# Windowed attention ahead of two MLPs: v loaded once in blocks by parity, attends two groups at a time, the first unit's k turned in banks of its own

## The chip, the cores and the metric

The kernel runs on one core of one Trainium2 chip. The metric is the device time of one execution in microseconds (us), lower is better. The time before is 992.86 us, the median of 3 runs (991.76 to 993.39).

## The reference

Three stages follow one another. The change touches only the first, causal attention over a window of 64 positions:

```python
# q, k, v: (4, 8, 576, 64) float32
scores = scale * q @ k^T                     # scale = 1/sqrt(64)
mask = (rel >= 0) & (rel < 64)               # rel = query position - key position
attn = softmax(where(mask, scores, -1e9))
x = (attn @ v) -> (2304, 512)                # heads side by side
x = gelu-like MLP: g = h * sigmoid(1.702 h), h = x @ w_in (512x2048), g @ w_out
out = top-2 of 8 experts by a noisy gate, each relu(x @ w1) @ w2, weighted sum
```

## The kernel before, in words

**Units and groups.** A unit is two heads of one batch entry; there are 16. A unit has 9 blocks of 64 queries. Each block sees 128 keys: the 64 of the block before and its own 64. Three blocks make a group, so a unit has 3 groups and the stage 48. A loop body handles two units, that is 6 groups, numbered m = 0 to 5. The first and the last body are written out, the six between are a hardware loop. The unit's parity (`par`) picks one of two buffers of qT, kT and v_pairs; the group's parity picks one of two PSUM banks for scores (`s_ps`), turned probabilities (`pt_ps`) and output (`o_ps`).

**Engines, each with its own fixed order.** The order of work is written out by hand for each engine, and semaphores join them. For group n, TensorE (PE) issues in this order: `turn_p(n-3)`, three transposes of normalised probabilities (L1509); `score(n)`, a mask product (L1498) and three products of queries and keys (L1501), each float32 product being two instruction records; `attend(n-4)`, six 64x64 products of probabilities and v, twelve records (L1523); after m = 0 and 3 six transposes of the next unit's q, after m = 1 and 4 six of its k (L1485). K is turned in batch 2 (four tiles) and batch 3 (two tiles), q in batches 0 and 1.

VectorE (DVE) takes the maximum (L1087, `nmx`), then for the group before it the sum (L1092, `dene`) and the reciprocal (L1095, `rden`), then copies the output of group n-5 (L1103), and it copies turned q (L1078) and k (L1081). ScalarE (ACT) copies turned probabilities (L853, `probT`), takes the exponentials (L861, `prob`) and copies turned q and k (L844, L847). GpSimd (POOL) multiplies by the reciprocal (L644, `norm`), which `turn_p` waits for, and in between converts MLP weights: `high_of_w` (L649) after m = 0 and 3, `low_of_w` (L654) after m = 1 and 4. At m = 2 and 5 it has the norm alone.

**Loads.** SyncE (SP) issues all loads in one order: v of this unit (L475, L476), q of the unit after the next (L464), weights (L481), k of the unit after the next (L470, four DMAs). `v_windows` reads 17 overlapping stretches of 128 rows, so that nearly every row of v arrives twice, and a last small DMA brings the first block's own half. V of unit u waits until unit u-2 is attended (`attended`); q waits until its single buffer is turned.

**Ends.** At the start PE turns q, then k of unit 0. All four batches go into halves of banks 3 and 4, so k batch 2 waits until DVE has copied q and k batch 3 until ACT has. At the end the last three groups are drained (`turn_p`, `attend` in turn), and the MLP begins (L1571) while its first inputs are still being split.

Of the kernel before, what the change touches and what calls it, by code (L numbers as in the profile page):

```python
# [11 lines left out]
P = 128  # L12
# [11 lines left out]
BLOCKS = S // QB  # L24
GB = 3
# [60 lines left out]
def build(nc, q, k, v, w_in, w_out, w_gate, w_noise, noise, w1, w2, out):  # L86
# [6 lines left out]
    v_v = v.rearrange("b (c two) (m p) d -> (b c) p (two m) d", two=2, p=QB)  # L93
    v_windows = bass.AP(v.tensor, v.offset, [[2 * S * DH, UNITS], [DH, P], [QB * DH, 2 * BLOCKS - 1], [1, DH]])
# [6 lines left out]
    with ctx:  # L101
# [28 lines left out]
        mask = sa("mask", [P, GB, P], mybir.dt.bfloat16)  # L130
# [5 lines left out]
        kT = [sa(f"kT{i}", [P, QB + S]) for i in range(2)]  # L136
# [150 lines left out]
        tr_ps = [banks[3][:, 0:S // 2], banks[4][:, 0:S // 2], banks[3][:, 0:SPLIT], banks[4][:, 0:S - SPLIT]]  # L287

# [24 lines left out]
        attended = sem("attended")  # L313
        o_copied = sem("o_copied")
# [139 lines left out]
        def k_part(u_par, batch):  # L454

            first = tiles_of(batch)[0] * TP
            count = len(tiles_of(batch)) * TP
            return kT[u_par][:, QB + first:QB + first + count], tr_ps[batch]

        @block.sync  # L460
        def _(sp):
# [148 lines left out]
        def _(pool):  # L610
# [5 lines left out]
            nc.gpsimd.memset(v_pairs[0][0:QB, 0, :], 0.0).then_inc(consts_ready, 1)  # L616
            nc.gpsimd.memset(v_pairs[1][0:QB, 0, :], 0.0).then_inc(consts_ready, 1)
            nc.gpsimd.memset(kT[0][:, 0:QB], 0.0).then_inc(consts_ready, 1)
            nc.gpsimd.memset(kT[1][:, 0:QB], 0.0).then_inc(consts_ready, 1)
            nc.gpsimd.memset(mask[:], 0.0).then_inc(consts_ready, 1)  # L620
            nc.gpsimd.memset(ident_b[:], 0.0).then_inc(consts_ready, 1)
            pool.wait_ge(consts_ready, 8)
            nc.gpsimd.affine_select(out=ident_b[:], in_=ident_b[:], compare_op=ALU.not_equal, fill=1.0, base=0,
                                    pattern=[[-1, P]], channel_multiplier=1).then_inc(consts_ready, 1)
            pool.wait_ge(consts_ready, 9)
            for h in range(2):
                half = mask[h * QB:(h + 1) * QB, :, :]

                nc.gpsimd.affine_select(out=half, in_=half, compare_op=ALU.is_gt, fill=NEG, base=0,
                                        pattern=[[0, GB], [1, P]], channel_multiplier=-1).then_inc(consts_ready, 1)  # L630
            pool.wait_ge(consts_ready, 11)
            for h in range(2):
                half = mask[h * QB:(h + 1) * QB, :, :]
                nc.gpsimd.affine_select(out=half, in_=half, compare_op=ALU.is_ge, fill=NEG, base=QB,
                                        pattern=[[0, GB], [-1, P]], channel_multiplier=1).then_inc(consts_ready, 1)
            pool.wait_ge(consts_ready, 13)

            nc.gpsimd.memset(mask[:, 0, 0:QB], NEG).then_inc(consts_ready, 1)
# [198 lines left out]
        def _(act):  # L837
            def turned(u, par, batch):
# [6 lines left out]
                else:  # L845
                    dst, src = k_part(par, batch)
                    ins = nc.scalar.activation(dst, src, ACT.Copy)  # L847
# [17 lines left out]
            def body(i, first, last):  # L865
                for m in range(6):
# [930 lines left out]
```

## Time and profile before

| | |
|---|---|
| median of the runs | 992.86 us |
| the profiled execution: its own time | 993.39 us |
| its span | 991.7 us |
| PE busy | 970.2 us (98%) |
| DVE, ACT, POOL busy | 546.6, 438.3, 484.2 us |
| queue q1 (all loads of SP) | 185.02 MB, 62.9% of 16 DMA engines |
| attention stage | from the start to the first MLP product at 116.59 us |

The device time of an execution lies about 1.7 us above its span. The page's share of busy time is an average over three different stages. A PE matmul's end is modelled, so the step from one start to the next tells more than the busy time. All times below are us from the span's start.

### The profile page before, as it was taken

The numbers are of one execution on the slowest core, as the hardware profiler recorded it, in microseconds if no ns is written. First come the engines' busy times: TensorE is split into PE (matmuls) and PEld (weight loads), VectorE is DVE, ScalarE is ACT, GpSimd is POOL, SyncE is SP. The second block draws the span as 40 slices with busy tenths as digits, with TensorE's granted clock in tenths as the row PEclk, the third lists the DMA queues.
The fourth block names the chain that finished last, engine by engine and source line by source line (L and its number), as shares of the span: only waits on it lengthen the run. The fifth ranks groups of instructions, "written<-read, shape, count | busy, mean of one in ns | idle before, by whom it ended". The sixth has DMA issues, their size and how long they took to land.

```text
span 991.7 us, 19802 instructions
## 1 busy us (share of the span) xinstructions
PE 970.2 (98%) x5432; PEld 844.7 (85%) x5433; DVE 546.6 (55%) x1328; ACT 438.3 (44%) x1094; POOL 484.2 (49%) x564
## 2 busy tenths in 40 slices
PE   7999999999999999999999999999999999999995
PEld 6888899999999999999998788888888888888884
DVE  4667622225225233243344887676777777767762
ACT  5899843333342342342243444443444444444431
POOL 5566678756877787787927221221221221122121
PEclk9999999999999999999999999999999999999998
DMA  7999677959999999999838525888976869494211
GB/s 176 213 220 221 122 232 257 319 166 309 341 294 328 321 316 338 318 286 291 267 114 290 175 85 160 253 268 274 258 224 207 254 181 292 135 283 140 55 57 49
DMA packets 252496, 225.25 MB, mean 227 GB/s; under 512 B 84620, under 2 KB 182412, under 8 KB 252432
## 3 DMA queue, kind: packets, MB, share of 16 engines
q1 hardware_dynamic: 214352, 185.02, 62.9%
q0 software_dynamic: 9280, 28.62, 8.1%
q10 hardware_dynamic: 28800, 10.83, 5.0%
q8 instruction: 32, 0.52, 0.2%
q14 instruction: 32, 0.26, 0.1%
HBM read 140.68 MB, written 85.82 MB: 228 GB/s over the span
## 4 chain that ended last, share of the span: by engine, by line
PE 94%; DVE 2%; DMA 2%; issue 1%; SPq 1%; ACT 1%; POOL 0%; POOLq 0%; ACTq 0%
PE bank L1674 22%; PE bank L1682 21%; PE bank L1571 20%; PE bank L1590 20%; PE bank L1501 3%; PE bank L1523 2%; PE bank L1485 2%; DMA q_raw<-q 2%; PE bank L1615 2%; PE bank L1509 1%; PE bank L1607 1%; DVE hT L1255 1%; PE bank L1498 1%; SPq L476 1%; DVE he L1274 0%
## 5 line engine op out<-in xcount | busy, mean ns | idle before, releaser
L1674 PE MATMUL bank<-W,xe 128*128 (+1 forms) x960 | 226.1, 391 | 0.0
L1682 PE MATMUL bank<-W,he 128*128 (+1 forms) x960 | 224.7, 389 | 1.1 <-DVE he L1274 1.1
L1674 PEld LDWEIGHTS bank<-W,xe 128*128 128x128 f32 x960 | 181.2, 189 | 37.8
L1682 PEld LDWEIGHTS bank<-W,he 128*128 128x128 f32 x960 | 179.9, 188 | 39.0 <-issue 1.9
L1590 PE MATMUL bank<-W,gs 128*128 128x512 f32 x864 | 205.8, 392 | 0.0
L1571 PE MATMUL bank<-xs,W 128*128 128x384 f32 x768 | 197.0, 337 | 0.2 <-DVE gs L1151 0.2
L1590 PEld LDWEIGHTS bank<-W,gs 128*128 128x128 f32 x864 | 161.2, 188 | 32.0
L1255 DVE STREAM_TRANSPOSE hT<-bank 32x256 f32<-32x256 f32 x320 | 144.1, 450 | 42.1 <-PE bank L1674 37.9
L1151 DVE TENSOR_TENSOR gs<-bank,gs 128x384 fp32r<-128x384 f32 x96 | 53.5, 557 | 187.2 <-ACT gs L900 187.2
L795 POOL DMA_INDIRECT out<-y_sb,yrow x40 | 41.3, 1032 | 233.5 <-DVE y_sb L1287 224.4
L958 ACT ACTIVATE hq<-bank 32x256 f32<-32x256 f32 x320 | 119.8, 374 | 67.2 <-PE bank L1674 61.4
L1571 PEld LDWEIGHTS bank<-xs,W 128*128 128x128 f32 x768 | 138.5, 188 | 3.0 <-DVE gs L1151 0.5
L900 ACT ACTIVATE gs<-bank 128x384 fp32r<-128x384 f32 x96 | 47.2, 492 | 200.2 <-PE bank L1590 194.4
L681 POOL TENSOR_TENSOR raw<-raw,xT 128x512 fp32r<-128x512 f32 x99 | 127.9, 1292 | 8.0
L1571 PE MATMUL bank<-xT_low,W 128*128 128x384 f32 x384 | 128.8, 335 | 0.0
L1330 DVE TENSOR_TENSOR bank<-bank,gate 128x384 f32<-128x384 f32 x96 | 53.9, 561 | 79.5 <-ACT gate L989 79.4
L679 POOL CAST xT<-raw 128x512 fp32r<-128x512 f32 x99 | 60.8, 614 | 45.8 <-DMA split_weights<-xT 45.2
L948 ACT ACTIVATE xe<-xr 128x512 fp32r<-128x512 f32 x40 | 25.3, 632 | 115.2 <-DVE xr L1234 115.2
L989 ACT ACTIVATE gate<-bank 128x384 f32<-128x384 f32 x96 | 47.0, 490 | 60.4 <-PE bank L1571 56.3
L1571 PEld LDWEIGHTS bank<-xT_low,W 128*128 128x128 f32 x384 | 72.1, 188 | 0.0
L784 POOL DMA_INDIRECT part<-out,yrow x40 | 42.8, 1071 | 46.6 <-issue 42.5
L1269 DVE SCALAR_TENSOR_TENSOR he<-hT,he 128x1024 fp32r<-128x1024 f32 x34 | 41.7, 1225 | 36.3 <-ACT he L971 36.3
(185 smaller groups left out, 1034.4 us busy)
## 6 DMA issues: line engine op xcount, KB each, us to landing
W<-split_weights SPq DMA_DIRECT2D x112, 512.0 KB
raw<-moe_w SPq DMA_DIRECT2D x128, 256.0 KB, 3.7
split_weights<-raw SPq DMA_DIRECT2D x112, 256.0 KB, 4.1
split_weights<-xT SPq DMA_DIRECT2D x99, 256.0 KB, 4.2
xg<-x_by_expert ACTq DMA_DIRECT2D x160, 64.0 KB
v_pairs<-v SPq DMA_DIRECT2D x16, 544.0 KB, 4.2
q_raw<-q SPq DMA_DIRECT2D x16, 288.0 KB, 3.7
out<-zeros SPq DMA_DIRECT2D x12, 384.0 KB, 4.5
```

The lines of the kernel that those rows point to most:

```text
L679: nc.gpsimd.tensor_copy(high_w, job_raw[n % 5]).then_inc(ej_high, 1)
L681: nc.gpsimd.tensor_tensor(low_w, job_raw[n % 5], high_w.bitcast(F32), ALU.subtract).then_inc(ej_low, 1)
L900: nc.scalar.activation(gs[c % 2][:, 0], h_ps[c % 2][:, 0:TG], ACT.Copy).then_inc(g_high, 1)
L958: ins = nc.scalar.activation(hq[c * Q:(c + 1) * Q, :].rearrange("p (k q i) -> p k q i", q=2, i=Q)[:, :, q], src[q * Q:(q + 1) * Q, :, c], ...
L989: nc.scalar.activation(gate[:], h_ps[c % 2][:, 0:TG], ACT.Sigmoid, scale=1.702).then_inc(sigmoided, 1)
L1151: nc.vector.tensor_tensor(gs[c % 2][:, 1], h_ps[c % 2][:, 0:TG], gs[c % 2][:, 0].bitcast(F32), ALU.subtract).then_inc(g_low, 1)
L1255: nc.vector.transpose(dst[c * Q:(c + 1) * Q, :, q], src[q * Q:(q + 1) * Q, :, c])
L1330: nc.vector.tensor_tensor(h_ps[c % 2][:, 0:TG], h_ps[c % 2][:, 0:TG], gate[:], ALU.mult).then_inc(gated, 1)
L1571: ins = nc.tensor.matmul(h_ps[c % 2][:, 0:TG], w_in_s[:, wl, c, d], x_low(g, d) if xl else x_high(g, d), start=(d == 0 and wl + xl == 0), ...
L1590: ins = nc.tensor.matmul(y_ps[t][:], gs[c % 2][:, gl, t * P:(t + 1) * P], w_out_s[:, wl, c], start=(c == 0 and gl + wl == 0), stop=(c == F ...
L1674: ins = nc.tensor.matmul(h2_ps[par][:, f * 512:(f + 1) * 512], xe[par][:, xl, d * P:(d + 1) * P], weights(e, wl, d * FE + f * 512), start= ...
L1682: ins = nc.tensor.matmul(ye_ps[par][:], he[par][:, hl, c * P:(c + 1) * P], weights(e, wl, W1COLS + c * DM), start=(c == 0 and wl + hl == 0 ...
```

## The change

Four parts. (1) V is read once, in four DMAs for a unit: for either head the even blocks into partitions 0 to 63 and the odd blocks into partitions 64 to 127. GpSimd then makes the missing halves with two copies for each unit (`pair_v`), after the norm of the unit's third group. In the loop the load of v now follows that of q. A window's key halves now stand even block first, and the mask and kT are laid out by parity to match; k's last batch becomes two copies on DVE. (2) PE attends groups n-5 and n-4 together at odd m instead of one at every m, and the first attend of a unit waits for `v_paired`. (3) K of unit 0 is turned into banks 5 and 6, and its two waits go. (4) ScalarE's table is loaded at the start of its stream.

```diff
@@ SyncE
-                sp.dma_start(v_pairs[par][:, 1:], v_windows[u]).then_inc(v_loaded[par], 16)
-                sp.dma_start(v_pairs[par][QB:P, 0:1], v_v[u, :, 0:1]).then_inc(v_loaded[par], 16)
+                for h in range(2):
+                    sp.dma_start(v_by_head(par, slice(0, QB))[:, h, 0:EVENS], v_even[u, :, h]).then_inc(v_loaded[par], 16)
+                    sp.dma_start(v_by_head(par, slice(QB, P))[:, h, EVENS:], v_odd[u, :, h]).then_inc(v_loaded[par], 16)
...
-                load_v(u, par)
+                if last or (isinstance(i, int) and i == 0):
+                    load_v(u, par)
                 if not last:
                     load_q(u + 2)
+                if not (last or (isinstance(i, int) and i == 0)):
+                    load_v(u, par)
@@ GpSimd
+            def pair_v(i, par):
+                pool.wait_ge(normed, i * 6 + par * 3 + 3)
+                pool.wait_ge(v_loaded[par], i * 64 + 64)
+                pool.sem_inc(v_seen, 1)
+                even, odd = v_by_head(par, slice(0, QB)), v_by_head(par, slice(QB, P))
+                nc.gpsimd.tensor_copy(even[:, :, EVENS:], even[:, :, 0:ODDS]).then_inc(v_paired, 1)
+                nc.gpsimd.tensor_copy(odd[:, :, 1:EVENS], odd[:, :, EVENS:]).then_inc(v_paired, 1)
+                pool.wait_ge(v_paired, i * 4 + par * 2 + 2)
...
                     norm(i * 6 + m, m)
+                    if m % 3 == 2:
+                        pair_v(i, m // 3)
@@ ScalarE and VectorE
-                    dst, src = k_part(par, batch)
+                    for dst, src in k_parts(u, par, batch):
...
+            nc.scalar.preload_act_table(ACT.Exp)
@@ TensorE
-                if batch == 2:
+                if batch == 2 and not first_unit(u):
                     pe.wait_ge(turned_dve, u * 2 + 1)
-                if batch == 3:
+                if batch == 3 and not first_unit(u):
                     pe.wait_ge(turned_act, u * 2 + 1)
...
-                    pe.wait_ge(v_loaded[par], i * 32 + 32)
+                    pe.wait_ge(v_paired, u * 2 + 2)
...
-                    if not (first and m < 4):
+                    if m % 2 and not (first and m < 5):
+                        attend(n - 5, i if m >= 5 else i - 1, (m - 5) % 6)
                         attend(n - 4, i if m >= 4 else i - 1, (m - 4) % 6)
```

On TensorE, before, m = 0 and m = 1 of the loop body hold one attend each. In the names prob, probT, kT, qT and v_pairs the digit is the buffer, and banks 3 and 4 take the turned q.

```order
L1498 MATMUL bank0<-mask,ident_b 128x384 [waits exped]
L1501 MATMUL bank0<-kT0,qT0 128x128 x3
L1523 MATMUL bank12<-probT0,v_pairs0 64x64 [waits o_copied]
L1523 MATMUL bank12<-probT0,v_pairs0 64x64 x5
L1485 MATMUL bank3<-ident,q_raw 128x96 [waits turned_act]
L1485 MATMUL bank4<-ident,q_raw 128x96 [waits turned_dve]
L1509 MATMUL bank56<-ident,prob1 128x128 [waits p_copied,normed]
L1498 MATMUL bank12<-mask,ident_b 128x384 [waits exped]
L1501 MATMUL bank12<-kT0,qT0 128x128 x3
L1523 MATMUL bank7<-probT1,v_pairs1 64x64 [waits o_copied,p_copied,v_loaded1]
```

The same place after the change, on TensorE: one stretch without attends, then both.

```order
L1547 MATMUL bank0<-mask,ident_b 128x384 [waits exped]
L1549 MATMUL bank0<-kT0,qT0 128x128 x3
L1534 MATMUL bank3<-ident,q_raw 128x96 [waits turned_act]
L1534 MATMUL bank4<-ident,q_raw 128x96 [waits turned_dve]
L1558 MATMUL bank56<-ident,prob1 128x128 x2
L1547 MATMUL bank12<-mask,ident_b 128x384 [waits exped]
L1549 MATMUL bank12<-kT0,qT0 128x128 x3
L1572 MATMUL bank12<-probT0,v_pairs0 64x64 [waits o_copied]
L1572 MATMUL bank12<-probT0,v_pairs0 64x64 x5
L1572 MATMUL bank7<-probT1,v_pairs1 64x64 [waits o_copied,p_copied,v_paired]
```

The attend of the odd unit's first group (v_pairs1) stands at the same m as before, but it now waits for GpSimd's copies, and the attend ahead of it came down from m = 0.

On GpSimd, before, the end of the loop body has three norms and no more than the weights' work between them.

```order
L644 TENSOR_TENSOR prob1<-prob1,rden 128x384 [waits exped,inverted]
L654 ISA [waits raw_high]
L654 TENSOR_TENSOR W<-w_raw1,W 128x512
L644 TENSOR_TENSOR prob2<-prob2,rden 128x384 [waits exped,inverted]
L664 COMPARE_AND_BRANCH
```

The same place after the change, on GpSimd:

```order
L678 TENSOR_TENSOR prob1<-prob1,rden 128x384 [waits exped,inverted]
L688 ISA [waits raw_high]
L688 TENSOR_TENSOR W<-w_raw1,W 128x512
L678 TENSOR_TENSOR prob2<-prob2,rden 128x384 [waits exped,inverted]
L696 COPY v_pairs1<-v_pairs1 64x2x256 [waits normed,v_loaded1]
L697 COPY v_pairs1<-v_pairs1 64x2x256
L710 REGISTER_ALU [waits v_paired]
L710 COMPARE_AND_BRANCH
```

The two copies stand behind the norm of m = 5, and the next body's first norm stands behind them.

## Rows read from the trace of the kernel before

**Rows 1.** Busy time by stretch: us, engines, granted clock, DMA share, GB/s.
```profile
50.00:75.00 25.00, 24.81 (x306) 22.43 (x305) 17.80 (x59) 22.48 (x92) 15.98 (x20) 1.00 1.04 221
```

**Rows 2.** Chain that ended last, 21 to 51 us: start, us, what.
```profile
21.46 0.48 PE bank L1509 x3
...
43.98 0.65 PE bank L1485 x6
...
45.12 0.67 PE bank L1501 x6
45.79 0.50 PE bank L1523 x12
46.29 0.64 PE bank L1485 x6
46.93 0.33 PE bank L1509 x3
...
50.40 0.68 PE bank L1485 x6
```

**Rows 3.** PE alone, one narrow window: start, us to the last record's end, count.
```profile
45.94 0.35 PE L1523 MATMUL bank<-probT,v_pairs 128*64 128x64 f32 x6
```

**Rows 4.** Who waits for whom, 25 to 105 us: total, times, longest.
```profile
PE bank L1485 <- DMA q_raw<-q: 1.7, 4, 0.8
```

**Rows 5.** The same for SP's DMA queue, 0 to 130 us.
```profile
SPq L475 <- PE bank L1523: 12.0, 12, 3.3
```

**Rows 6.** All engines in order of time, a piece of one loop body.
```profile
45.30 0.87 ACT L844 ACTIVATE qT<-bank 64x288 f32<-64x288 f32 x2
...
46.19 0.49 ACT L853 ACTIVATE probT<-bank 128x384 f32<-128x384 f32 x1
...
48.90 0.33 PE L1498 MATMUL bank<-mask,ident_b 128*128 128x384 bf16 x1
50.02 0.56 DVE L1087 TENSOR_REDUCE nmx<-bank 128x3 f32<-128x384 f32 x1 [0.53 <-PE bank L1501]
50.50 0.15 DVE L1092 TENSOR_REDUCE dene<-den 128x3 f32<-128x6 f32 x1
51.06 0.83 POOL L644 TENSOR_TENSOR prob<-prob,rden 128x384 f32<-128x384 f32 x1
```

**Rows 7.** The conversion L649, 20 to 106 us: ns min/median/max.
```profile
L649 POOL CAST W<-w_raw x14: 609/612/614, 20.1 to 105.8; 128x512 f32 x12, 128x512 fp32r<-128x512 f32 x2
```

**Rows 8.** All engines in order of time, the start.
```profile
3.02 1.10 POOL L629 TENSOR_SCALAR_AFFINE_SELECT mask<-mask 64x384 bf16<-64x384 bf16 x2
4.27 1.10 POOL L634 TENSOR_SCALAR_AFFINE_SELECT mask<-mask 64x384 bf16<-64x384 bf16 x2
4.42 1.19 PE L1485 MATMUL bank<-ident,q_raw 96*128 96x96 f32 x6 [4.42 <-DMA q_raw<-q]
5.70 1.28 ACT L844 ACT_TABLE_LOAD   x1 [5.54 <-PE bank L1485]
...
8.58 0.36 DVE L1081 COPY kT<-bank 128x192 f32<-128x192 f32 x1 [2.40 <-PE bank L1485]
9.08 0.48 PE L1498 MATMUL bank<-mask,ident_b 128*128 128x384 bf16 x1 [0.54 <-DVE kT L1081]
```

**Rows 9.** All engines in order of time, the end of the stage.
```profile
112.24 0.55 PE L1509 MATMUL bank<-ident,prob 128*128 128x128 f32 x3
112.44 0.37 ACT L861 ACTIVATE prob<-bank,nmx 128x128 f32<-128x128 f32 x1 [0.27 <-DVE nmx L1087]
114.08 0.83 POOL L644 TENSOR_TENSOR prob<-prob,rden 128x384 f32<-128x384 f32 x1 [0.49 <-DVE rden L1095]
114.39 0.57 PE L1523 MATMUL bank<-probT,v_pairs 128*64 128x64 f32 x12 [0.20 <-DVE xT L1103]
114.96 0.55 PE L1509 MATMUL bank<-ident,prob 128*128 128x128 f32 x3
116.59 0.62 PE L1571 MATMUL bank<-xs,W 128*128 128x384 f32 x2
```

More of the change, by code:

```diff
@@ L135, in build @@
         qT = [sa(f"qT{i}", [P, BLOCKS, 2, QB]) for i in range(2)]
-        kT = [sa(f"kT{i}", [P, QB + S]) for i in range(2)]
+        kT = [sa(f"kT{i}", [P, 2, EVENS, QB]) for i in range(2)]
         v_pairs = [sa(f"v_pairs{i}", [P, 2 * BLOCKS, DH]) for i in range(2)]
@@ L313, in build @@
         attended = sem("attended")
+        v_paired = sem("v_paired")
+        v_seen = sem("v_seen")
+        v_zero = sem("v_zero")
         o_copied = sem("o_copied")
@@ L452, in q_parts, with first_unit, turned_bank, k_parts @@
                        tr_ps[h][e * DH:(e + 1) * DH].rearrange("c (b p) -> c b p", b=BLOCKS))
[L454 to L458, printed above, removed]
+        def first_unit(u):
+            return isinstance(u, int) and u == 0
+        def turned_bank(u, batch):
+            return (first_tr_ps if first_unit(u) else tr_ps)[batch]
+        def k_parts(u, u_par, batch):
+            src = turned_bank(u, batch)
+            if batch == 2:
+                half = SPLIT // QB // 2
+                yield kT[u_par][:, :, 0:half], src.rearrange("c (j e k) -> c e j k", e=2, k=QB)
+            else:
+                blocks = src.rearrange("c (n k) -> c n k", k=QB)
+                first = SPLIT // QB
+                yield kT[u_par][:, 0, first // 2:EVENS], blocks[:, 0:BLOCKS - first:2]
+                yield kT[u_par][:, 1, first // 2:ODDS], blocks[:, 1:BLOCKS - first:2]
+        def k_window(u_par, qb):
+            view = kT[u_par][:].rearrange("c e j k -> c (e j) k")
+            j = qb // 2
+            other = EVENS + (j if qb % 2 else (j - 1) % EVENS)
+            return view[:, j:other + 1:other - j]
+        def v_slot(h, qb):
+            return h * BLOCKS + (EVENS if qb % 2 else 0) + qb // 2
+        def v_by_head(u_par, rows):
+            return v_pairs[u_par][rows].rearrange("p (h s) d -> p h s d", h=2)
         @block.sync
@@ L626, in _ @@
             for h in range(2):
[L627 to L635, printed above, removed]
@@ L636, in _ @@
-            pool.wait_ge(consts_ready, 13)
-            nc.gpsimd.memset(mask[:, 0, 0:QB], NEG).then_inc(consts_ready, 1)
+                half = mask[h * QB:(h + 1) * QB].rearrange("q s (b k) -> q (s b) k", k=QB)
+                for at in (0, 3):
+                    nc.gpsimd.affine_select(out=half[:, at::4], in_=half[:, at::4], compare_op=ALU.is_ge, fill=NEG, base=0,
+                                            pattern=[[0, 3 - at // 3], [-1, QB]], channel_multiplier=1).then_inc(consts_ready, 1)
@@ L640, in norm @@
+                for at in (2, 5):
+                    nc.gpsimd.affine_select(out=half[:, at::4], in_=half[:, at::4], compare_op=ALU.is_gt, fill=NEG, base=0,
+                                            pattern=[[0, 2], [1, QB]], channel_multiplier=-1).then_inc(consts_ready, 1)
+            pool.wait_ge(consts_ready, 15)
+            nc.gpsimd.memset(mask[:, 0, QB:P], NEG).then_inc(consts_ready, 1)
             def norm(n, m):
@@ L1079, in turned @@
                 else:
-                    dst, src = k_part(par, batch)
-                    ins = nc.vector.tensor_copy(dst, src)
+                    for dst, src in k_parts(u, par, batch):
+                        ins = nc.vector.tensor_copy(dst, src)
                 ins.then_inc(turned_dve, 1)
@@ L1127, in _ @@
             ins.then_inc(q_zero, 1)
+            for par in range(2):
+                nc.vector.memset(v_by_head(par, slice(QB, P))[:, :, 0], 0.0).then_inc(v_zero, 1)
             dve.wait_ge(q_zero, 1)
@@ L1496, in score @@
                 bank = s_ps[(par * 3 + g) % 2]
-                allowed = mask[:] if g == 0 else mask[:, 1:2, :].to_broadcast([P, GB, P])
+                allowed = mask[:, g:g + GB]
                 nc.tensor.matmul(bank[:, 0:GB * P], ident_b[:], allowed, start=True, stop=False)
                 for b in range(GB):
-                    at = (g * GB + b) * QB
-                    ins = nc.tensor.matmul(bank[:, b * P:(b + 1) * P], qT[par][:, g * GB + b].rearrange("c h q -> c (h q)"),
-                                           kT[par][:, at:at + P], start=False, stop=(b == GB - 1))
+                    ins = nc.tensor.matmul(bank[:, b * P:(b + 1) * P].rearrange("q (n k) -> q n k", n=2),
+                                           qT[par][:, g * GB + b].rearrange("c h q -> c (h q)"),
+                                           k_window(par, g * GB + b), start=False, stop=(b == GB - 1))
                 ins.then_inc(scored, 1)
```

28 lines of the change are left out of this document (15 added, 13 removed).

## The prediction

> **What bounds the kernel now.** I read the page first: the change touches only the attention stage, the first 116.6 us of the span, where the first MLP product starts [rows 9]. Then the busy time by stretch. From 50 to 75 us TensorE is busy for 24.81 of 25 us at full granted clock, ScalarE for 22.48, VectorE for 17.80, GpSimd for 15.98, and the DMA share is 1.04 [rows 1]. Two resources look full, so the chain and the waits must tell them apart. The chain is TensorE instruction after instruction: the reader should see that each piece begins where the last one ends, score 0.67, attend 0.50, six transposes 0.65, three transposes 0.33 [rows 2]. In 80 us TensorE waited 1.7 us for q, four times, 0.8 at most [rows 4], while SyncE waited 12.0 us for TensorE's attends before it could load v [rows 5]. So the loads are paced by TensorE, and TensorE bounds, with the loads just behind.
>
> One step from one turning of q to the next is 43.98 to 50.40, 6.42 us [rows 2], a body of two units 12.85. From the first `turn_p` of body 1 (21.46 [rows 2]) to the first one of the drain (112.24 [rows 9]) are 90.8 us; the last body lacks one turning of q and one of k, 1.15 by the chain's 0.65 and 0.50, so a body took (90.8 + 1.15) / 7 = 13.13. The 0.28 above 12.85 are waits, those for q above all.
>
> **Attends in pairs.** Three transposes take 0.48 behind an attend at 21.46 [rows 2] and 0.33 behind six transposes [rows 2]: leaving an attend costs 0.15. Twelve records of an attend take 0.50 [rows 2], but in the stream six of them end after 0.35 with 0.22 of that the last one's length [rows 3], so a step is about 0.027 and twelve need 0.31 to 0.35: entering costs 0.15 too. A second attend right behind the first thus costs 0.35, and a pair saves 0.30. Three pairs in a body save 0.90: 12.85 becomes 11.95 if nothing else is late. This is work off the critical engine, so it counts in full unless a wait eats it. The waits for q should go as well, since v is now 1152 rows of 256 bytes for a unit instead of 2240, of some 4530 in all four loads.
>
> **The new wait, in the loop.** What is late next? GpSimd's pair of copies. The attend of an odd unit's first group stands at m = 1, the second of its pair, and waits for `v_paired`; the copies stand behind the norm of m = 5 of the body before. Take the mask product of m = 0 as zero. Before, that norm began 51.06 - 48.90 = 2.16 later, because VectorE sums only after the maximum of m = 0 (50.02, 50.50) [rows 6]. It takes 0.83, so it ends at 2.99. The copies wait for it; a GpSimd instruction that waits for GpSimd's own last one began 0.15 late (3.02 + 1.10 = 4.12, next 4.27) [rows 8]. No row shows a copy of 64 partitions by 512 elements. The nearest is the conversion of 128 by 512, 0.61 [rows 7]; two, slightly overlapped, 1.2. With 0.05 for the semaphore v is ready at 4.4. TensorE would come to that attend at 0.16 + 0.67 + 0.50 (q) + 0.33 + 0.16 + 0.67 + 0.50 (first attend) = 2.99. It waits 1.4 us, and behind it in its queue stand the turning of k, the next `turn_p` and the next score, so all is late by that. The bounds of one copy: 0.31 if half the partitions took half the time of rows 7, and 1.11 if it ran at the norm's rate (0.83 for 384 elements [rows 6]); over two copies and seven bodies and the drain, 16 copies, that is -4.8 and +8.0 us. I take 0.61, the same operation with the same elements for each partition.
>
> The even unit's pair stands behind the norm of m = 2, and its attend is the first of m = 5, almost three steps later; I find it ready some 0.7 before and cost it at nothing. GpSimd has the room: 15.98 of 25 is 8.4 in a body, and 2.4 are added. The norm of m = 0 and m = 3 starts behind the copies, and `turn_p` wants it three groups later; also nothing, but with little over.
>
> The Trainium skill speaks to this cover: its page "GPSIMD Engine Reference", section 1, says that GpSimd shares its SBUF interfaces with VectorE and contends with it in some of its modes. Fourteen conversions took 609 to 614 ns while VectorE was busy for 71% of the time [rows 1, 7], so this trace shows no such stretch; by the rule the copies would be longer and the time higher.
>
> **A smaller wait.** At odd m the copy of probT on ScalarE now waits for the first attend of the same m, which ends about 1.5 behind the mask (0.16 + 0.67 + 0.57 [rows 2, 9] and the entry). Copy (0.4 of its 0.49), exponentials (1.2) and q (0.87) [rows 6] bring ScalarE's q to 4.0; TensorE wants it for k batch 3 at m = 4, at 0.83 + 0.85 + 0.65 + 0.33 + 0.83 + 0.33 = 3.8. Cost 0.2 for a body, between 0 and 0.4. At m = 1 the long wait covers it. The second DVE copy of k (some 0.25 for a unit) lies in VectorE's idle third.
>
> So a body is 11.95 + 1.4 + 0.2 = 13.55, and the seven, less 1.25 for what the last lacks (0.2 of it the small wait, the rest the two turnings without a full exit), 93.6 against 90.8: +2.8.
>
> **The start.** Before, ScalarE loads its table only when the first q is turned (5.70, 1.28 us), k waits for q's copies, and the first mask product starts at 9.08 [rows 8]. Now TensorE turns q until 5.6 and k right behind at the same pace, 0.2 each, until 6.8. VectorE copies k in two pieces until 7.5 (the whole took 0.36 [rows 8]), ScalarE's q and k end near 7.0. The mask product starts at 7.5, 1.5 earlier. The mask's constants took 1.10 for two pieces of 384 [rows 8]; eight pieces of 128 to 192 are ready between 5.5 and 7.5. The next q and k are loaded no earlier by as much, so I take 1.35, between 0.8 and 1.7.
>
> **The drain.** The last pair of copies stands behind the very last norm, and TensorE wants it one attend earlier, before `turn_p(47)`. From `turn_p(45)` (112.24) the norm began at 1.84, the attend at 2.15 and the MLP at 4.35 [rows 9]. Exponentials and `turn_p(45)` both move by about 0.3, so the norm still starts near 1.8 and ends at 2.6; copies until 3.95; the attend starts at 4.0, then `turn_p(47)` and the rest as before. That is +1.85, between +1.2 and +2.9 by the copies' bounds.
>
> **The sum.** -1.35 + 2.8 + 1.85 = +3.3 us. Against the profiled execution's 993.39 this is 996.7, against the median 996.2; I say 996.4.
>
> **Rivals.** (A) The copies are hidden: GpSimd has 9 idle us for every 25 [rows 1], and if the norm ran earlier than I think, all of the pairing's gain stays. Bodies 7 x 11.95 - 1.05 = 82.6, that is -8.2, with the start and no loss in the drain: -9.5, 983.5. Against it: the norm cannot start before VectorE's sum, 1.6 behind the mask [rows 6], and so v not before 3.8. Chance 0.10.
> (B) The loads bound the stage: share 1.04 [rows 1]. Then the waits of the loop are theirs, 24% fewer packets take 13.13 to 10.0, below TensorE's 11.95, and TensorE waits for copies as in A only where its lead allows; about 985. SyncE's 12.0 us of waiting [rows 5] speaks against it. Chance 0.04. The Trainium skill would back it: "DMA: Bandwidth & Descriptors", Specifications, wants 512 bytes for a transfer at line rate, and v's and k's rows here have 256; but the trace has TensorE wait only 1.7 us of 80, so the rule, true or not, prices nothing large.
> (C) The other side of my size: the copies run at the two-input rate. +8.0 more, 1004.4, slower. It decides from some 0.9 us a copy, where also GpSimd (8.4 + 3.6 + waits of 13.5) begins to hold `turn_p`. Chance 0.06.
> (D) The copies are near 0.35: the wait is 0.85, the sum -0.9 at 0.35 each, 992; or TensorE wastes less than I count at one of 23 pairs. Within 0.2% or faster. Chance 0.22. A late k (for the even unit v, weights and k stand behind the attend of m = 1; 0.8 was the longest wait for a load [rows 4]) would fall beside the wait for v and not add to it.
>
> The forecast has 0.58. A measurement of this kernel can tell 0.2% (2 us) from no change. Faster: A, B and 0.09 of D, 0.23. Same: 0.13 of D and 0.06 of the forecast, 0.19. Slower: the rest of the forecast and C, 0.58. The range is 989.5 to 1001; A, B and C lie outside.
>
> **What would show it.** `v_paired` from GpSimd's L697 as the longest releaser of TensorE's attends (L1572), about 1.4 at m = 1 of each body, none at m = 5; the copies 0.61 each; 7.5 for the first mask product; six transposes at m = 0 straight behind the score, 12 records at a second attend in 0.35; a DMA share near 0.8 and no wait for q. I am wrong if TensorE's attends never wait for GpSimd, or if the body is under 13.

## The result: 1001.48 us, 0.9% slower

The changed kernel takes 1001.48 us (median of 5 runs, 1000.35 to 1001.88), the kernel before 992.38 (991.76 to 993.39) beside it: ratio 1.0089, interval 1.0079 to 1.0100. The forecast was 996.4 with a range to 1001.0, so the direction was right and the size was not: +9.1 us instead of +4.

The profiled execution has a span of 1000.2 us against 991.7. The first MLP product starts at 125.25 instead of 116.59 [rows 9], 8.66 later, and what lies behind it takes 874.95 instead of 875.1. The loss lies in the attention stage, as far as these two traces show it.

### The profile page after: what moved, and what is told of

Same layout as the page of the kernel before. It is cut to its first block, busy times and chain, and to the rows that moved or that the text cites. A ratio compares the mean times of both kernels' runs of the same rounds, so it can differ in the third digit from the quotient of the medians.

```text
span 1000.2 us, 19972 instructions
## 1 busy us (share of the span) xinstructions
PE 967.8 (97%) x5432; PEld 844.7 (84%) x5433; DVE 546.4 (55%) x1346; ACT 439.4 (44%) x1094; POOL 502.9 (50%) x598
## 4 chain that ended last, share of the span: by engine, by line
PE 91%; DVE 2%; issue 2%; POOL 1%; SPq 1%; DMA 1%; ACT 1%; POOLq 0%; DVEq 0%; ACTq 0%
PE bank L1725 21%; PE bank L1733 21%; PE bank L1622 20%; PE bank L1641 20%; PE bank L1549 2%; PE bank L1572 2%; PE bank L1666 2%; PE bank L1534 1%; PE bank L1558 1%; PE bank L1658 1%; DVE hT L1304 1%; POOL prob L678 1%; DMA k_raw<-k 1%; PE bank L1547 1%; POOL v_pairs L697 0%
```

## The profile after

First the start of the stage, all engines in order of time (start, us, instruction, in brackets the wait before it and who ended it).

```profile
4.40 1.19 PE L1534 MATMUL bank<-ident,q_raw 96*128 96x96 f32 x6 [4.40 <-DMA q_raw<-q]
5.38 1.17 PE L1534 MATMUL bank<-ident,k_raw 96*128 96x96 f32 x6
...
6.59 0.42 DVE L1128 COPY kT<-bank 128x128 f32<-128x128 f32 x2 [0.43 <-PE bank L1534]
...
7.37 0.48 PE L1547 MATMUL bank<-mask,ident_b 128*128 128x384 bf16 x1 [0.82 <-ACT kT L893]
```

K is turned straight behind q, and the first mask product stands at 7.37 instead of 9.08 [rows 8]. Now who waits for whom from 25 to 105 us (total, times, longest), first TensorE, which has these two lines alone, then SyncE's queue from 0 to 130 us.

```profile
PE bank L1572 <- POOL v_pairs L697: 7.9, 6, 1.3
PE bank L1534 <- DMA k_raw<-k: 1.2, 2, 0.8
```

```profile
SPq L499 <- PE bank L1534: 5.6, 7, 1.8
...
SPq L511 <- PE bank L1572: 2.9, 3, 1.3
```

The waits for q [rows 4] are gone, and TensorE's attends wait for GpSimd's copies once in each of the six bodies. SyncE, which used to wait 12.0 us for attends before it could load v [rows 5], waits 2.9. Over the loop alone, from 25 to 105 us, the whole of SyncE's waiting is one line, first before, then after:

```profile
SPq L475 <- PE bank L1523: 7.0, 10, 1.2
```

```profile
SPq L499 <- PE bank L1534: 1.5, 4, 0.6
```

The queue of loads has lost most of its slack. The next fence says why: the v_pairs tile over the whole stage, ns min/median/max of one.

```profile
L511 SPq DMA_DIRECT2D v_pairs<-v x32: 595/618/861, 8.2 to 115.0; - x32
L512 SPq DMA_DIRECT2D v_pairs<-v x32: 598/607/631, 9.0 to 115.7; - x32
...
L696 POOL COPY v_pairs<-v_pairs x16: 602/602/687, 17.3 to 120.7; 64x512 f32<-64x512 f32 x16
L697 POOL COPY v_pairs<-v_pairs x16: 608/612/613, 17.9 to 121.4; 64x512 f32<-64x512 f32 x16
```

A copy takes 0.60 to 0.61 (one of the 32, in the drain, 0.69). V's four DMAs hold SyncE for some 0.6 us each; before, one of 0.39 and one of 1.55 did for the unit.

One piece of a loop body, in order of time:

```profile
49.10 0.33 PE L1547 MATMUL bank<-mask,ident_b 128*128 128x384 bf16 x1
...
51.22 0.83 POOL L678 TENSOR_TENSOR prob<-prob,rden 128x384 f32<-128x384 f32 x1 [0.20 <-DVE rden L1142]
...
51.68 0.57 PE L1572 MATMUL bank<-probT,v_pairs 128*64 128x64 f32 x12
...
52.24 0.60 POOL L696 COPY v_pairs<-v_pairs 64x512 f32<-64x512 f32 x1 [0.19 <-POOL prob L678]
...
52.83 0.63 SPq L511 DMA_DIRECT2D v_pairs<-v  x1
52.90 0.61 POOL L697 COPY v_pairs<-v_pairs 64x512 f32<-64x512 f32 x1
...
53.57 0.57 PE L1572 MATMUL bank<-probT,v_pairs 128*64 128x64 f32 x12 [1.32 <-POOL v_pairs L697]
...
54.07 0.71 PE L1534 MATMUL bank<-ident,k_raw 96*128 96x96 f32 x6
...
57.03 1.10 PE L1572 MATMUL bank<-probT,v_pairs 128*64 128x64 f32 x24
57.05 0.36 DVE L1150 COPY xT<-bank 128x192 f32 x1 [0.24 <-issue]
```

Read it from the mask product at 49.10. The norm starts 2.12 later, the copies 3.14, v is ready at 4.41, and TensorE's second attend starts at 4.47. Note also SyncE at 52.83: the even unit's next v is issued when the first attend of the pair is done, before the wait ends. The end of the stage:

```profile
117.86 0.55 PE L1558 MATMUL bank<-ident,prob 128*128 128x128 f32 x3
...
119.65 0.83 POOL L678 TENSOR_TENSOR prob<-prob,rden 128x384 f32<-128x384 f32 x1 [0.51 <-DVE rden L1142]
...
121.42 0.61 POOL L697 COPY v_pairs<-v_pairs 64x512 f32<-64x512 f32 x1
122.09 0.91 PE L1572 MATMUL bank<-probT,v_pairs 128*64 128x64 f32 x12 [2.34 <-POOL v_pairs L697]
...
123.76 1.56 PE L1572 MATMUL bank<-probT,v_pairs 128*64 128x64 f32 x24
...
125.25 1.01 PE L1622 MATMUL bank<-xs,W 128*128 128x384 f32 x2
```

And busy time by stretch (us, busy time and count for PE, PEld, DVE, ACT, POOL; granted clock, DMA share, GB/s):

```profile
50.00:75.00 25.00, 22.03 (x273) 20.20 (x272) 16.64 (x58) 21.07 (x84) 18.96 (x25) 1.00 0.67 168
120.00:124.00 4.00, 1.91 (x19) 1.47 (x21) 1.72 (x4) 0.89 (x3) 1.78 (x3) 0.65 0.29 68
124.00:128.00 4.00, 4.00 (x33) 3.88 (x32) 1.56 (x4) 2.46 (x4) 2.35 (x9) 0.50 0.26 72
```

TensorE falls from 24.81 busy of 25 to 22.03, the DMA share from 1.04 to 0.67 [rows 1]. And where TensorE waited 2.34 us for the last copies, its granted clock then lies at 0.50, the lower of its two levels: the pair of attends at 123.76 takes 1.56, where the same pair takes 1.22 in e5 below, at a granted clock of 1.00.

| From the traces, us | before | after | difference | forecast |
|---|---|---|---|---|
| start to the mask product of m = 0 of body 1 | 21.78 | 20.51 | -1.27 | -1.35 |
| from there to `turn_p(45)` | 90.46 | 97.35 | +6.89 | +2.8 |
| `turn_p(45)` to the first MLP product | 4.35 | 7.39 | +3.04 | +1.85 |
| sum | 116.59 | 125.25 | +8.66 | +3.3 |

## The experiments

"Body" is a third of the time from the mask product at m = 0 of body 4 to that of body 7. The wait is TensorE's longest sum from 25 to 105 us, with its releaser. A body's mean moves between traces of one loop by up to 0.5 (e13 and e14 differ in the last unit alone). Each run was timed beside the kernel before, whose median was 991.6 to 992.8 in these groups (the first row has the one of the result above), so small differences between two rows are better taken from the ratios. "Start" stands for parts 3 and 4 of the change, "pairs" for part 2, "two k DMAs" for k of a unit in two DMAs.

| run | median us | ratio to before, interval | body | longest sum of waits | MLP at |
|---|---|---|---|---|---|
| before | 992.4 | | 13.01 | q 1.7 | 116.59 |
| after | 1001.48 | 1.0089, 1.0079 to 1.0100 | 13.90 | copies 7.9 | 125.25 |
| e1: start | 990.24 | 0.9976, 0.9965 to 0.9987 | 12.84 | q 1.2 | 113.98 |
| e2: pairs | 1006.0 | 1.0143, 1.0121 to 1.0165 | 15.68 | q 10.6 | 130.91 |
| e3: after, single attends | 1013.19 | 1.0219, 1.0198 to 1.0240 | 15.43 | copies 13.6 | 135.58 |
| e4: after, copies a group earlier | 999.99 | 1.0075, 1.0056 to 1.0095 | 13.85 | k 7.8 | 124.57 |
| e8: the odd unit's alone | 999.21 | 1.0063, 1.0047 to 1.0080 | 13.73 | k 7.1 | 124.01 |
| e5: after, last unit without copies | 999.84 | 1.0074, 1.0057 to 1.0091 | 13.97 | copies 6.6 | 123.02 |
| e6: after, half the copies | 1000.12 | 1.0078, 1.0061 to 1.0095 | 13.69 | copies 4.5, k 2.7 | 123.03 |
| e7: windows, start, pairs, q first | 993.89 | 1.0017, 1.0004 to 1.0029 | 13.32 | k 5.1 | 119.80 |
| e9: e4, two k DMAs | 996.81 | 1.0059, 1.0040 to 1.0079 | 13.37 | k 4.8 | 121.34 |
| e10: e7, two k DMAs | 991.9 | 0.9995, 0.9980 to 1.0010 | 12.80 | k 4.4 | 116.39 |
| e11: e1, two k DMAs | 989.86 | 0.9983, 0.9973 to 0.9993 | 12.91 | q 0.6 | 114.17 |
| e12: after, two k DMAs | 1000.02 | 1.0086, 1.0069 to 1.0103 | 13.79 | copies 7.9 | 123.02 |
| e13: e8, two k DMAs, k ahead of v | 997.33 | 1.0059, 1.0043 to 1.0076 | 13.87 | norms 2.4, copies 2.3 | 120.65 |
| e14: e13, last unit as in e5 | 996.85 | 1.0053, 1.0037 to 1.0070 | 13.35 | norms 2.9 | 119.43 |
| e15: e10, k ahead of v | 993.23 | 1.0015, 1.0003 to 1.0028 | 13.10 | k 3.8 | 116.46 |

### The parts alone: e1_start, e2_group, e3_ungroup

e1 is the kernel before with the start's edits; e2 is the kernel before with the pairs; e3 is the changed kernel with single attends.

```diff
@@ e1_start (against before)
-            return kT[u_par][:, QB + first:QB + first + count], tr_ps[batch]
+            return kT[u_par][:, QB + first:QB + first + count], turned_bank(u, batch)
...
+            nc.scalar.preload_act_table(ACT.Exp)
...
-                if batch == 2:
+                if batch == 2 and not first_unit(u):
@@ e2_group (against before)
-                    if not (first and m < 4):
+                    if m % 2 and not (first and m < 5):
+                        attend(n - 5, i if m >= 5 else i - 1, (m - 5) % 6)
                         attend(n - 4, i if m >= 4 else i - 1, (m - 4) % 6)
@@ e3_ungroup (against after)
-                    if m % 2 and not (first and m < 5):
-                        attend(n - 5, i if m >= 5 else i - 1, (m - 5) % 6)
+                    if not (first and m < 4):
```

Expected of e1:

> The kernel before with the start alone: k of unit 0 in banks 5 and 6, its two waits gone, ScalarE's table loaded first. My theory: the first mask product comes 1.5 us earlier (about 7.5 instead of 9.08), body 1 starts 1.3 earlier, and since TensorE bounds the loop it stays: -1.3 us, ratio 0.9987. Rival, that the loads bound the loop: they catch up in the first bodies and the gain is lost, 0 us.

Measured: the first mask product at 7.02, 2.06 earlier than before, and 2.1 us less, somewhat more than expected. The start's edits are a gain by themselves; which of the two brings it was not tried.

Expected of e2:

> The kernel before with the attends in pairs alone, v loaded as before by overlapping windows. If TensorE alone bounds the loop a body goes from 13.1 to about 12.3 us (0.90 saved, 0.2 lost on ScalarE's q): -5 us. Rival, the loads: their packets took 102.8% of 16 engines at 6.45 us a unit, so that a body cannot get much under 12.8 us, and TensorE waits for q or k instead: -2 us at most, waits for DMA up by 0.5 us a body.

Measured: 13.6 us slower, the worst single part. TensorE alone, then SyncE's queue, in the same piece of a body:

```profile
47.61 1.21 PE L1485 MATMUL bank<-ident,q_raw 96*128 96x96 f32 x6 [2.05 <-DMA q_raw<-q]
...
49.26 0.53 PE L1498 MATMUL bank<-mask,ident_b 128*128 128x384 bf16 x1
49.58 1.49 PE L1501 MATMUL bank<-kT,qT 128*128 128x128 f32 x6
```

```profile
47.00 0.39 SPq L475 DMA_DIRECT2D v_pairs<-v  x1
47.48 1.92 SPq L476 DMA_DIRECT2D v_pairs<-v  x1
...
49.71 0.33 SPq L464 DMA_DIRECT2D q_raw<-q  x1
```

The second DMA of v is followed by q, so q waits on SyncE until v may be loaded, and v may only when the later attend is done. The six products of a score behind the 2.05 us of waiting take 1.49 instead of the 0.83 that they take elsewhere: here too the clock is at its lower level for a while. So q ahead of v, which the change has too, is what keeps the pairs from costing 13.6; e7 below, with that order, confirms it.

Expected of e3:

> The changed kernel with one attend at every m again; v once, the copies and the start stay. My theory: the odd unit's first attend still waits for GpSimd's copies, 1.2 instead of 1.47 us, the re-entry behind the wait and the 0.2 of the small waits at m = 3 and 4 go, the 0.90 of the pairs is lost: a body near 14.0 as with pairs, so the time is that of the changed kernel within 1.5 us (1001.5). Rival, that the pairs are what costs: 995 or less.

Measured: 11.7 slower than the changed kernel. My expectation had forgotten a second wait. With single attends the even unit's first attend stands at m = 4 instead of m = 5, before its copies are done, so both units wait: 11 waits in place of 6. The pairs are worth having once the copies are there.

### Taking the copies' wait away: e4_swap, e8_swap_odd, e6_half_copy

e4 puts `pair_v` before `low_of_w` for both units; e8 for the odd unit only; e6 copies only head 0's halves from the third unit on, so a part of attention is not computed.

```diff
@@ e4_swap (against after)
-                pool.wait_ge(normed, i * 6 + par * 3 + 3)
+                pool.wait_ge(normed, i * 6 + par * 3 + 2)
...
-                    if m % 3 == 2:
+                    if m % 3 == 1:
                         pair_v(i, m // 3)
...
-                    if m % 3 == 1 and not (last and m == 4):
+                    if m % 3 == 2 and not (last and m == 5):
@@ e8_swap_odd (against after)
-                    if m % 3 == 2:
+                    if m in (2, 4):
                         pair_v(i, m // 3)
...
-                    if m % 3 == 1 and not (last and m == 4):
+                    if m in (1, 5) and not (last and m == 5):
@@ e6_half_copy (against after)
-                nc.gpsimd.tensor_copy(even[:, :, EVENS:], even[:, :, 0:ODDS]).then_inc(v_paired, 1)
+                h = slice(0, 2) if isinstance(i, int) and i == 0 else slice(0, 1)
+                nc.gpsimd.tensor_copy(even[:, h, EVENS:], even[:, h, 0:ODDS]).then_inc(v_paired, 1)
```

> The changed kernel with the places of two GpSimd steps exchanged: the copies of v behind the norm of m = 1 and 4, the weights' second conversion behind that of m = 2 and 5. The odd unit's copies then end about 1.2 to 2.5 us earlier and TensorE's attend at m = 1 waits 0 to 0.3 instead of 1.4; the last unit's copies lie before the last norm. My theory, that this wait with what follows from it is the loss: a body of 12.2 to 12.6, the drain back to 4.4 us without the fall of TensorE's clock, in all -10 to -13 against the changed kernel, 988 to 992, at or under the kernel before. Rival, that v lands too late there or that GpSimd is full: the norm waits behind it, 997 or more.

> The changed kernel with the odd unit's copies alone moved one norm ahead (behind m = 4) and its weights' conversion behind m = 5; the even unit's stay behind m = 2. In the full exchange v of the even unit came late and k waited 7.8 us behind it in all. My theory: v of the odd unit has landed by then or lands within 1.4 us, TensorE waits 0.1 to 0.5 at m = 1 instead of 1.3, the drain has no wait for copies and no fall of the clock: a body of 12.7 to 13.0, -9 to -11 against the changed kernel, 990.5 to 992.5, about the kernel before. Rival, that k's loads fill the gap at m = 4: 995 or more, with waits for k of 0.8 us a body.

> The changed kernel with each of GpSimd's two copies half as long from the third unit on: only the first head's half blocks are copied, the second head keeps what the first units left (that part of the attention isn't computed). My theory: each copy 0.34 instead of 0.61, v ready 0.5 earlier, so the wait at m = 1 goes from 1.3 to 0.8, seven bodies and the drain: -4 to -4.5 us against the changed kernel, 997. Rival, that the loads (SyncE issues v for 3.1 us a unit) would then hold TensorE: -2 us, with waits for k up by 0.3 us a body.

Measured: 1.5, 2.3 and 1.4 us less than after, where 1.5 us of waiting in each of seven bodies could have come back; all three missed what was expected and ended at their rivals. In e6 a copy takes 0.39 to 0.40, the waits for copies in the loop fall to 0.9 each and those for k rise to 2.7 in all; the wait in the drain is still 2.17. In the loops of e4 and e8 the attends no longer wait for GpSimd. What waits instead stands in TensorE's line of e4 from 25 to 105 us:

```profile
PE bank L1534 <- DMA k_raw<-k: 7.8, 7, 2.0
```

Its cause is on SyncE's queue, e4, and then on TensorE:

```profile
53.89 0.63 SPq L511 DMA_DIRECT2D v_pairs<-v  x1
54.71 0.61 SPq L512 DMA_DIRECT2D v_pairs<-v  x1
55.50 0.60 SPq L511 DMA_DIRECT2D v_pairs<-v  x1
56.28 0.60 SPq L512 DMA_DIRECT2D v_pairs<-v  x1
57.08 0.45 SPq L517 DMA_DIRECT2D w_raw<-moe_w_in  x1
57.72 1.90 SPq L505 DMA_DIRECT2D k_raw<-k  x4
```

```profile
53.06 0.96 PE L1572 MATMUL bank<-probT,v_pairs 128*64 128x64 f32 x24
...
61.27 0.55 PE L1534 MATMUL bank<-ident,k_raw 96*128 96x96 f32 x4 [1.03 <-DMA k_raw<-k]
62.21 0.38 PE L1534 MATMUL bank<-ident,k_raw 96*128 96x96 f32 x2 [0.39 <-DMA k_raw<-k]
```

The attend at m = 1 lets v go at 53.89; v's four issues stand 0.8 apart, then come the weights and four of k, until 59.6, and k has landed at 61.2, when TensorE has stood for 1.03. So there are two limits, one on the other: the copies, and beneath them the even unit's chain attend, v, w, k. In the changed kernel they lie side by side, as the prediction said of a late k, because v is issued at the first attend of the pair, ahead of the wait. Each alone holds a body near 13.8 (13.79 with the copies alone, e12 below; 13.85 and 13.73 with k alone, e4 and e8), which is why lifting the first gave nearly nothing.

Something smaller comes up as well. From the mask product of m = 1 to the next are 2.94 to 3.02 us in e4's full bodies and from there to that of m = 3 1.33 to 1.48, where the forecast's steps are 2.66 and 1.15; e7 and e9 have the same. A part is TensorE's wait for VectorE's copy of q (0.9 us in five waits in e4), the rest was not followed. So even with copies and k on time a body here would take about 12.4 by these steps, not 11.95.

The drain is not free of the copies in either. In e4 the attend of the last unit's first group waits 0.92 for them, and a turning in the last body 1.51 for a norm. For e8 no wait and no fall of the clock were expected; its attend waits as follows, and the clock falls to 0.50 behind it:

```profile
120.78 0.57 PE L1572 MATMUL bank<-probT,v_pairs 128*64 128x64 f32 x12 [1.33 <-POOL v_pairs L697]
```

### The drain: e5_last_dma

The last unit's v is loaded whole by eight DMAs, and its attends wait for them instead of for copies.

```diff
+                    if isinstance(u, int) and u == UNITS - 1:
+                        sp.dma_start(v_by_head(par, slice(0, QB))[:, h, EVENS:], v_even[u, :, h, 0:ODDS]).then_inc(v_loaded[par], 16)
+                        sp.dma_start(v_by_head(par, slice(QB, P))[:, h, 1:EVENS], v_odd[u, :, h]).then_inc(v_loaded[par], 16)
```

> The changed kernel, but the last unit's v comes wholly by DMA (eight DMAs instead of four) and GpSimd copies nothing for it. Only the drain differs. In the changed kernel TensorE waited 2.3 us in the drain for the last pair of copies and its granted clock fell to 0.5 from about 122 to 128 us. My theory: both go, 2.1 from the wait and 0.9 to 1.3 from the clock, -3.2 us against the changed kernel (998.3). Rival, that another wait of the drain takes the place (the last norm): -1.5 or less, the clock still falling.

Measured: from `turn_p(45)` to the MLP 4.89 us instead of 7.39, and 1.6 us less in the runs, half of the 3.2 expected. The attend now waits 0.88 for v's DMA, and the clock stays up in the same windows as above:

```profile
120.00:124.00 4.00, 3.04 (x46) 2.58 (x46) 3.43 (x9) 3.02 (x7) 1.58 (x9) 1.00 0.24 28
124.00:128.00 4.00, 3.78 (x22) 3.46 (x22) 1.33 (x3) 2.50 (x5) 1.86 (x3) 1.00 0.53 142
```

So without the copies the long wait and the lower clock are both gone here. That it is the wait and not the copies that counts, e14 below shows: it has no copies there either, but its attend waits 1.58 for v's DMA, and the clock falls to 0.50. What the lower clock costs can be read from e12, whose drain has the same wait as after's, while its clock falls only about when the MLP begins:

```profile
120.83 0.57 PE L1568 MATMUL bank<-probT,v_pairs 128*64 128x64 f32 x12 [2.33 <-POOL v_pairs L693]
```

```profile
118.00:122.00 4.00, 1.67 (x24) 1.19 (x26) 2.16 (x7) 1.58 (x5) 2.13 (x3) 1.00 0.36 71
```

From this attend to the MLP are 2.19 us, in after 3.16.

### The chain of loads: e7_windows, e9_swap_k2, e10_windows_k2, e11_start_k2, e12_after_k2

e7 is the kernel before with start, pairs and q ahead of v, so without copies. The four others load k of a unit in two DMAs, ahead of w, and TensorE waits for k once a unit:

```diff
@@ two k DMAs (e9 to e15)
-                after(sp, qk_turned, u * 4 + batch - 3)
-                t = slice(0, T0) if batch == 2 else slice(T0, TT)
+                after(sp, qk_turned, u * 4)
                 for h in range(2):
-                    sp.dma_start(k_raw[:, t, h * DH:(h + 1) * DH], k_v[u, h, :, t, :]).then_inc(k_loaded[batch - 2], 16)
+                    sp.dma_start(k_raw[:, :, h * DH:(h + 1) * DH], k_v[u, h]).then_inc(k_loaded[0], 16)
...
-                if not (last and par):
-                    load_w(i + par, 1 - par)
                 if not last:
                     load_k(u + 2, 2)
-                    load_k(u + 2, 3)
+                if not (last and par):
+                    load_w(i + par, 1 - par)
```

> The kernel before with attends in pairs and the start, and the load of v behind that of q, as in the changed kernel; v still comes twice, by overlapping windows, with no copies. The first trial of pairs alone lost 12.6 us of waits for q, which stood in SyncE's queue behind a v that had to wait for the pair at m = 1. If that order was the whole trouble, the waits for q go and a body takes 12.2 to 12.6 us: 985 to 988 (-5 to -8 against before). Rival, that the loads bound it (1.0 of the DMA engines' time at 6.45 us a unit): a body stays at 12.8 or more, with waits for k or q of 0.4 us or more each, 990 or more.

> The changed kernel with the copies of a pair of tiles ahead of low_of_w's casts for both units (as the earlier run with that order), and with k of a unit loaded by two DMAs (one a head, six tiles) in place of four, issued ahead of w as soon as both k batches are turned. Theory (under the copies' wait lies the even unit's chain of loads v, w, k on SP's queue): SP's k issues shrink from 2.0 us to about 1.0 and start 0.55 earlier, so the wait of k's turn at m=4 falls from 1.0-1.5 us to 0-0.4, a body comes to 12.4-13.0 and the time to 989-993. Rival (the DMA engines themselves are full and the fewer issues change nothing): body 13.8 as with the order alone, 999.

> The kernel before with the first unit's banks, the attends of two groups together, q ahead of v in SP's order, and k of a unit in two DMAs ahead of w; v by windows as before, so no copies by GpSimd. Theory (chain of loads on SP): the k wait of the run without the merged k (5.1 us in 5 waits) goes, body 12.2-12.9, time 983-988. Rival (windows move more bytes and the DMA engines' share is 1.0 already): body stays at or above 12.8 or k lands late still, 989 or more.

> The kernel before with the first unit's banks and the early table load, and k of a unit in two DMAs ahead of w; attends one group at a time as before. Theory: there PE sets the pace (bodies of 12.83, k never late), so the merged k changes nothing: 990.2 within 1. Rival (loads set the pace there too): 987 or less.

> The changed kernel with only k of a unit in two DMAs ahead of w. Theory (the copies' wait at m=1 comes first and the k chain lies beneath it): the copies' wait of 1.3 us stays, only the few k waits go; body 13.9 to 13.7, 1000-1001. Rival (the k chain is the main limit by itself): 995 or less.

Measured: e7 has no copies and still bodies of 13.3, with 5.1 us of waiting for k. That is 7.6 us less than after, and 3.7 more than e1: even without copies the pairs lose more to the loads than they save. e12 is as expected (copies 7.9 as in after, 1000.0; the two late k of after are gone) and e11 too (0.4 less than e1, within the intervals): where TensorE sets the pace or the copies come first, k's issues cost little. e9 gained on e4, 3.2 by the medians and 1.6 by the ratios, but k is still waited for, 4.8 us, and a wait of 2.40 for a norm comes in its last body; the expected 989 to 993 was missed, since k is issued behind v's 3.2 us all the same. e10 gained 2.0 on e7 and came out at the time of before, at the upper rival, 2.0 above e11, which has single attends. SyncE waits 13.3 us of the 80 for TensorE there, so its queue is not full as a whole; but its issues of v (ns min/median/max) are long, the second of a unit up to 4027 ns, where before 1977 was the most.

```profile
L483 SPq DMA_DIRECT2D v_pairs<-v x16: 368/389/510, 8.0 to 108.3; - x16
L484 SPq DMA_DIRECT2D v_pairs<-v x16: 1486/2020/4027, 8.5 to 108.7; - x16
```

### The order of the queue: e13_kfirst, e14_kfirst_last, e15_windows_kfirst

For the even unit of the loop k now stands ahead of v; e13 has e8's order of copies, e14 adds e5's edit, e15 is e10 with k first.

```diff
@@ against the kernels with two k DMAs
+                ahead = par == 0 and not last and not isinstance(i, int)
+                if ahead:
+                    load_k(u + 2, 2)
                 if not (last or (isinstance(i, int) and i == 0)):
                     load_v(u, par)
-                if not last:
+                if not (last or ahead):
                     load_k(u + 2, 2)
```

> The changed kernel with the odd unit's pair of copies one group earlier, k of a unit in two DMAs, and for the even unit k issued ahead of v. If SP's queue order is the second limit, k lands some 3 us earlier and its wait at m=4 (1.0 us with the merged k alone) goes: body 12.2 to 12.8, waits for k under 1 us in 80, time 989 to 993. If the DMA engines are the limit, the body stays near 13.5 and the time at 997. A third way: v, now 1.1 later, is late for GpSimd's copies, and PE waits for v_pairs at m=5 instead: 995 or more.

> The same with the last unit's v loaded whole by eight DMAs and no copies for it, so the drain has no wait for GpSimd. From the earlier run of this edit alone (drain 4.9 us in place of 7.4, 1.7 us of the time): 2 us under the run without it, 987 to 991, at or below the kernel before. If the drain were already short there (the odd pair stands one group earlier), within 0.7 of it.

> The kernel before with the first unit's banks, attends in pairs, q ahead of v, merged k, and for the even unit k ahead of v; v by windows, no copies. If only SP's order holds it: no k wait, body 12.2, 984 to 987. If the loads' bytes are the limit (a window DMA held SP's queue for 1.7 to 4.0 us of issue in the run before, with the DMA share at 1.0): the body stays at 12.7 to 13.0 and the time at 990 to 992, whatever the order.

Measured: e13 ended on its third way. Its waits from 25 to 105 us, three lines over all engines and one of TensorE's own:

```profile
POOL v_pairs L695 <- DMA v_pairs<-v: 12.1, 10, 2.0
...
PE bank L1557 <- POOL prob L677: 2.4, 7, 0.6
PE bank L1571 <- POOL v_pairs L696: 2.3, 4, 1.1
```

```profile
PE bank L1533 <- DMA k_raw<-k: 0.3, 1, 0.3
```

The wait for k is gone (0.3 us), and v is late instead: GpSimd stands 12.1 us waiting for it, its norms with it, and TensorE waits for norms and copies. With the same bytes and a DMA share of 0.65 to 0.74 the wait moved with the order of the queue. That speaks for the chain of issue and landing on SyncE's queue as the limit of this kernel, and against the bytes; a second queue would prove it and was not tried. e14 gained 0.5, within the interval, against 2 expected; its drain takes 5.93, with the wait of 1.58 for v's DMA and the lower clock named above. e15 is no better than e10: there the share is 1.06 to 1.09 from 50 to 100 us, and the order does not help.

No combination beat e1 and e11. These two beat both kernels, by some 2 us against before (ratios 0.9976 and 0.9983) and over 11 against after.

## Why the prediction was off

**Start: right.** -1.27 against -1.35; the mask product stood at 7.37 where 7.5 was said.

**What the pairs save: right where nothing waits.** From the mask product of m = 5 over the next body's to its m = 1 are 2.15 + 1.66 = 3.81 us, before 1.80 + 2.30, so a pair saves 0.30. Taken from the steps without a wait a body adds up to 11.95, as forecast, but no run has such a body: the shortest in the loop with pairs takes 12.73 (e10), and about 0.5 of that is the small waits which come up at m = 1 and 2 when the copies are on time. The waits for q are gone.

**The copies: right, place and size.** 0.60 and 0.61 against 0.61; the norm at 2.12 (2.16 said); v ready at 4.41 (4.4 said); a wait of 1.32 (1.4 said), in the loop at m = 1 only. The 0.05 for the semaphore had no row behind it; here the attend starts 0.06 behind the copy's end. The copies of the loop did not stretch with VectorE busy for 67% of the time. The Trainium skill, "GPSIMD Engine Reference", section 1, says that the two engines contend for SBUF in some of their modes; this trace shows no such case. Rival C and most of D fall with that.

**The body: the failed step.** "So a body is 11.95 + 1.4 + 0.2 = 13.55" came out at 13.87 in a body without other waits, and the seven went from 90.46 to 97.35, +6.89 instead of +2.8. The terms missing from it, about 4.1 in all:
- The pair that is split by a wait is a pair no longer. The second attend enters the stream anew: from its start (53.57) to k's turning (54.07) are 0.50, where 0.35 was counted. 0.15 a body, about 1.0 in seven. The saving of the pairing and its wait were added as if they were independent.
- At m = 3 the second attend of a pair finds its output bank not yet copied: the pair at 57.03 takes 1.10 instead of 0.92, and VectorE's copy ends at 57.41. 0.17 a body, 1.0 in six (the last body's pair at 112.73 takes 0.92). The forecast looked at the probT copy at odd m (0.2 said, 0.21 measured at m = 4) and not at the output's.
- K late in two bodies, 14.72 and 14.19 instead of 13.87: 1.2. In the others a late k did lie beside the wait for the copies, as said.
- The last body, where `turn_p` at 115.49 waits 0.53 for a norm, and small steps: some 0.9, by difference.

**The drain: mechanism right, a term missing.** The attend came 4.23 behind `turn_p(45)` (4.0 said). Behind it "the rest as before" took 3.16 instead of 2.20, because TensorE ran at its lower clock (0.50) behind a wait of 2.34 us; in e12 the same stretch at full clock takes 2.19. That is 1.0 of the 1.2 missed. The profiled execution may be the costlier one in this: its mean granted clock is 0.992, that of the other four 0.994, as in e12's profiled one.

**Rival A was priced wrongly, and that is the larger lesson.** 983.5 was to follow if the copies were hidden. e4 and e8 hid them in the loop, and the time was 1000 and 999. SyncE's v issues were left without a price, although they went from about 2.0 to 3.0 us a unit (50.60 to 52.62 before, 53.89 to 56.88 in e4), and with them the chain behind an attend: v, weights, k, landing. Its 12.0 us of waiting [rows 5] was read as slack of the loads; but that wait was for an event which the pairing itself makes later, and the issues ate the rest.

What stays open: the 0.4 us between the sums of the trace (+8.66, span +8.5) and the medians (+9.1), which is within the spread of the runs; and whether v on another engine's queue would free the pairs' saving, which was not tried.

## What to carry to other kernels

Before you price the wait that a change adds, ask which limit lies directly beneath it: price the whole chain from the event that frees a buffer through every issue on the queue to the landing, for otherwise "if it were hidden" is a number for a kernel that does not exist. Putting work together only saves its entries if both halves are ready at once; a wait between them gives the saving back. And where a wait on TensorE comes near 2 us, or falls into a stretch that is already broken by waits, allow for a lower clock behind it, about 1 us here.

## What the runs showed of the hardware

A DMA of 64 partitions with rows of 256 bytes held SyncE 0.60 to 0.62 us, now and then longer (0.86 at most in after), and the next stood 0.8 behind its start (53.89, 54.71, 55.50), although the DMA engines were free for a third of the time. One issue of a v window took up to 4.03 us in e10 and 1.98 at most before, with the DMA share near or above 1 in both. A GpSimd copy that depends on the norm before it began 0.19 to 0.26 behind its end.

TensorE's granted clock fell to 0.50 behind a wait of 1.85 us (e8), of 2.00 to 2.05 (e2 three times, e4) and of 2.17 to 2.40 (e6, e7, e9, e12, after and, in the drain, e3). It stayed at 1.00 behind the others of the loop, up to 1.67 (e2) and 1.80 (e3), and behind 1.51 (e4). But in the drain it fell behind shorter ones too, 1.33 (e8, e13) and 1.58 (e14), where TensorE had been busy for 0.4 to 0.7 of each of the two microseconds before. So the length of the last wait alone does not tell; and for the same wait it came while the wait still ran (after, within the microsecond from 121) or some 2 us behind its end (e12).
